# Layer-one routing with 8-column counting products, fused steps from threshold to list, and a different share of expert work per round

## What is computed

```python
def _moe_ref(x, w_gate, w1, w2):
    N, D = x.shape                       # 3072 tokens, 512 features
    E = w_gate.shape[1]                  # 8 experts
    cap = N // E                         # 384 tokens each
    logits = x @ w_gate
    order = np.argsort(-logits.flatten())
    assigned = -np.ones(N, dtype=np.int64)
    counts = np.zeros(E, dtype=np.int64)
    for idx in order:                    # best (token, expert) pair first
        tok, e = (int(idx) // E, int(idx) % E)
        if assigned[tok] >= 0 or counts[e] >= cap:
            continue
        assigned[tok] = e
        counts[e] += 1
...
    for e in range(E):
        mask = assigned == e
        h = np.maximum(x[mask] @ w1[e], 0.0)     # w1[e]: 512 x 1024
        out[mask] = h @ w2[e]                    # w2[e]: 1024 x 512
```

## Time and profile before

| | us |
|---|---|
| median of 3 runs | 844.89 |
| lowest and highest | 844.82, 845.41 |
| profiled execution | 845.31 |
| its span | 843.5 |

### The profile page before, as it was taken

One profiled execution on the slowest core, in us unless ns is written; L12 is line 12 of the kernel. 1 busy time (PEld: TensorE's weight loads), 2 busy tenths in 40 slices (PEclk: granted clock), 3 DMA queues, 4 the chain that ended last, 5 costly groups with the idle time before them and its releaser, 6 DMA issues.

```text
span 843.5 us, 15049 instructions
## 1 busy us (share of the span) xinstructions
PE 797.3 (95%) x4960; PEld 510.3 (61%) x4960; DVE 465.2 (55%) x2146; ACT 228.2 (27%) x681; POOL 216.0 (26%) x313
## 2 busy tenths in 40 slices
PE   5999997797899999999999999999999999999996
PEld 5878785786345445454554545555577686777762
DVE  6989895677777676776767677607049100000000
ACT  5878785421102121121211212121111111110101
POOL 6888973001021020302102021120300321211110
PEclk9999999899999999999999999999999999999999
DMA  9976650436071440706225071446987999898983
GB/s 260 279 235 208 222 151 2 181 129 224 6 262 51 142 170 3 283 26 222 90 75 211 26 261 51 148 164 240 361 321 293 414 372 348 308 338 310 332 318 105
DMA packets 64506, 171.66 MB, mean 204 GB/s; under 512 B 5585, under 2 KB 5585, under 8 KB 64449
## 3 DMA queue, kind: packets, MB, share of 16 engines
q1 hardware_dynamic: 54512, 143.70, 48.3%
q0 software_dynamic: 6480, 20.91, 6.8%
q10 hardware_dynamic: 3456, 6.29, 1.9%
HBM read 148.41 MB, written 22.81 MB: 203 GB/s over the span
## 4 chain that ended last, share of the span: by engine, by line
PE 75%; DVE 14%; DMA 4%; issue 3%; POOL 3%; ACT 1%; DVEq 0%; SPq 0%; POOLq 0%; ACTq 0%
PE bank L1433 16%; PE bank L1447 16%; PE bank L1575 11%; PE bank L1557 11%; DVE junk L987 4%; PE bank L1301 4%; PE bank L1328 3%; PE bank L1310 3%; PE bank L1506 2%; DMA weights<-in_moe_w 1%; PE bank L1298 1%; PE bank L1422 1%; PE bank L1633 1%; PE bank L1601 1%; PE bank L1646 1%
## 5 line engine op out<-in xcount | busy, mean ns | idle before, releaser
L1433 PE MATMUL bank<-features,weights 128*128 128x384 f32 x512 | 182.3, 497 | 0.6 <-ACT features L749 0.6
L1447 PE MATMUL bank<-weights 128*128 128x512 f32 x384 | 179.2, 602 | 0.0
L987 DVE TENSOR_SCALAR_CACHE_REDUCE junk<-Vt,cand 128x192 bf16<-128x192 f32 x376 | 136.1, 410 | 4.8
L1433 PEld LDWEIGHTS bank<-features,weights 128*128 128x128 f32 x512 | 89.5, 191 | 50.6 <-issue 5.6
L1557 PEld LDWEIGHTS bank<-x2T,weights 128*128 128x128 f32 x896 | 102.2, 192 | 5.9 <-issue 5.9
L1557 PE MATMUL bank<-x2T,weights 128*128 128x128 f32 x896 | 102.6, 275 | 0.0
L1447 PEld LDWEIGHTS bank<-weights 128*128 128x128 f32 x384 | 66.8, 190 | 58.5 <-issue 56.5
L1575 PE MATMUL bank<-weights,h2T 128*128 128x512 f32 x224 | 98.8, 593 | 0.4 <-ACT h2T L816 0.4
L1147 DVE SCALAR_TENSOR_TENSOR o<-bank,gate,x 128x512 f32<-128x512 f32 x14 | 10.5, 751 | 154.5 <-PE bank L1575 154.4
L754 ACT ACTIVATE weights<-bank 128x384 f32<-128x384 f32 x64 | 31.4, 490 | 141.4 <-PE bank L1433 141.4
L1575 PEld LDWEIGHTS bank<-weights,h2T 128*128 128x128 f32 x224 | 41.3, 190 | 46.5 <-issue 46.5
(11 more groups left out here) (324 smaller groups left out, 1048.3 us busy)
## 6 DMA issues: line engine op xcount, KB each, us to landing
weights<-in_moe_w SPq DMA_DIRECT2D x52, 2048.0 KB, 9.6
vw<-in_vwin SPq DMA_DIRECT2D x16, 576.0 KB, 4.9
qc<-in_qT SPq DMA_DIRECT2D x16, 384.0 KB, 5.3
kc<-in_kT SPq DMA_DIRECT2D x16, 384.0 KB, 5.8
vc<-in_vT SPq DMA_DIRECT2D x16, 384.0 KB, 7.4
x_rows<-xr SPq DMA_DIRECT2D x24, 256.0 KB, 2.2
y_rows<-weights ACTq DMA_DIRECT2D x24, 256.0 KB
weights<-x_rows,gidx POOLq DMA_INDIRECT x24
```

The source lines that it names most:

```text
L987: ins = ve.tensor_scalar(junk[:, c, :], Vt[:, :], cand[:, c:c + 1].bitcast(fp32), 0.0, ALU.is_ge, ALU.add, accum_out=cnt[:, c:c + 1])
L1433: ins = mm(HB[r % 2][:, 0:CAP], w1[:, c, 128 * r:128 * r + 128], xgT[:, c, :], start=(c == 0), stop=(c == KC - 1))
L1447: ins = mm(YB[j % 2][:, :], hT[:, r, 128 * j:128 * j + 128], w2[:, r, :], start=(r == 0), stop=(r == FC - 1))
```

## The change

- **Narrow products.** The count product streams the 8 columns of cnt, where it streamed them 16 times over (128). The threshold product streams 8 columns, the base products 2. The two base products now accumulate into one result of two columns (rowt has a zero column ahead, so that the second one is shifted), where VectorE added two results.
- **Fewer steps from threshold to list.** The comparison with tau and the multiply by revE are one step, the comparison with oneM and the multiply by V another. The steps to e_i move behind the row copy. The part of the rank that does not need the base is made before the base product is waited for, and the base is read as a scalar out of PSUM. The comparison that leaves oneE as a mask moves behind sel.
- **The first list's copies move ahead.** In search(1) alone, folded is copied before the first comparison and gidx right after it.
- **A signal for each tile.** xg_in becomes xg_in0 to xg_in2. TensorE waits for a tile's own.
- **Window 1's table.** The rounds get 111 units (6 in the second round, then 9, 6, 6 five times) where they got 90, the step behind the threshold product 16 for 15, the step behind the base product 22 for 28: 161 units for 145. The other windows' tables are as before.

```diff
@@ first_max @@
                 o.step(ve.tensor_reduce(m, src, X, ALU.max))
+                first_list = isinstance(ids_of, int) and ids_of == 0
+                if first_list:
+                    fold_out(ids_of)
                 o.step(ve.tensor_tensor(tmp, src, bc(m, shape, 2), ALU.is_equal))
-                if ids_of is not None:
+                if first_list:
+                    ids_out(ids_of)
+                elif ids_of is not None:
                     fold_out(ids_of)
...
-                if ids_of is not None:
+                if ids_of is not None and not first_list:
                     ids_out(ids_of)
@@ search @@
-                o.step(ve.tensor_scalar(oneE[:, :], TAU[:, 0:E], tau[:, :], None, ALU.is_equal))
-                o.step(ve.tensor_tensor(oneE[:, :], oneE[:, :], revE[:, :], ALU.mult))
+                o.step(ve.scalar_tensor_tensor(out=oneE[:, :], in0=TAU, scalar=tau[:, :], in1=revE[:, :],
+                                               op0=ALU.is_equal, op1=ALU.mult))
                 o.step(ve.tensor_reduce(oneM[:, :], oneE[:, :], X, ALU.max))
-                o.step(ve.tensor_scalar(oneE[:, :], oneE[:, :], oneM[:, :], None, ALU.is_equal))
+                o.step(ve.scalar_tensor_tensor(out=t1[:, :, :], in0=bc(oneE[:, :], full, 1), scalar=oneM[:, :], in1=V[:, :, :],
+                                               op0=ALU.is_equal, op1=ALU.mult))
+                o.step(ve.tensor_reduce(mx[:, :], t1[:, :, :], X, ALU.add))
...
+                ve.tensor_copy(rowt[:, 1:3], scn[:, :, NT - 1]).then_inc(s["rows_ready"], 1)
+                o.step(ve.scalar_tensor_tensor(out=rank[:, :, :], in0=scn[:, :, :], scalar=float(-BIG_SLOT), in1=GT[:, :, :],
+                                               op0=ALU.add, op1=ALU.subtract))
                 o.step(ve.tensor_scalar(e_f[:, :], oneM[:, :], -1.0, float(E), ALU.mult, ALU.add))
...
+                dve.wait_ge(s["base_mm"], ph + 1)
                 for h in range(2):
-                o.step(ve.tensor_copy(base[:, 0:2], BAS[:, 0:2]))
-                o.step(ve.tensor_copy(base[:, 2:3], BASN[:, 0:1]))
-                o.step(ve.tensor_tensor(base[:, 1:2], base[:, 1:2], base[:, 2:3], ALU.add))
...
+                    o.step(ve.scalar_tensor_tensor(out=rank[:, h, :], in0=rank[:, h, :], scalar=BAS[:, h:h + 1],
                                                    in1=GT[:, h, :], op0=ALU.add, op1=ALU.mult))
...
                 o.step(ve.tensor_scalar(sel[:, :], slot[:, :], CAP - 0.5, None, ALU.is_lt))
+                o.step(ve.tensor_scalar(oneE[:, :], oneE[:, :], oneM[:, :], None, ALU.is_equal))
@@ room @@
                 if w == 1:
-                    return [0] + [0, 0, 6] + [6] * (ROUNDS - 3) + [15, 28, 4, 8]
+                    return [0] + [0, 6] + [9, 6, 6] * 5 + [16, 22, 4, 8]
@@ load_x @@
-                if j == 0:
-                    pe.wait_ge(s["xg_in"], 16 * CT * (k + 1))
+                pe.wait_ge(s[f"xg_in{j}"], 16 * (k + 1))
@@ window @@
-                    mm(CNT, same_e[:, :], cnt[:, :].unsqueeze(1).to_broadcast([128, WIDE // 8, 8]),
-                       start=True, stop=True).then_inc(s["cnt_mm"], 1)
+                    mm(CNT, same_e[:, :], cnt[:, :], start=True, stop=True).then_inc(s["cnt_mm"], 1)
...
-                mm(BAS, tri[:, :], rowt[:, :], start=True, stop=True)
-                mm(BASN, ones_bf[:, :], rowt[:, :], start=True, stop=True).then_inc(s["base_mm"], 1)
+                mm(BAS, tri[:, :], rowt[:, 1:3], start=True, stop=False)
+                mm(BAS, ones_bf[:, :], rowt[:, 0:2], start=False, stop=True).then_inc(s["base_mm"], 1)
```

45 lines of the change are left out of this document (21 added, 24 removed).

## The result

The kernel before took 845.15 us beside it, the changed kernel 858.81 us (medians of four runs each): a ratio of 1.0154, 95% interval 1.0124 to 1.0183. I had predicted 841.5 us and a range of 838.5 to 844.4. The profiled execution took 857.25 us with a span of 855.4, 11.9 us more than the 843.5 of before.

A forecast was written before the change was run, and what follows sets the result against it. TensorE was taken as the bound (75% of the chain of waits, VectorE 14%). Windows 0, 1 and 2 gain 1.2, 3.25 and 0.7, windows 3 to 7 lose 1.75: 844.89 - 3.4 gives 841.5 us, range 838.5 to 844.4.

The forecast's parts named there:

- rival (c): Windows 3 to 7: gather of x, asked for earlier, lands 1.0 us late each (846.5) or 1.3 (848.0); chance 7%.
- 1.3 us in hand: Windows 3 to 7: gather lands 3.7 us after issue, so 1.3 us remain before the first tile of x is used.
- No wait for it shows before: Layer one's gather of x: argument against lateness, as the kernel before shows no wait for it.
- rival (b): Regrouping costs what it brings: 0.65 us lost in each of windows 3 to 7, window 1's fold later; 844.0; chance 12%.
- the expert's number 1 us later: Window 0, behind tau: number comes 1 us later, weights still have 5 us in hand with ten for 2 MB.
- The regrouping: Windows 3 to 7: 16 shifted units make more rounds short; 0.35 us lost per window, 1.75 in five.
- +0.2 with 16 units more: Window 1: takes 161 units, not 145, yet lasts only 0.2 us longer, saving later windows 3.45 us of products.
- 25.5 us to the threshold product: Window 1, from count 3 (9.9 us after V) to the threshold product: 25.5 us, where it was 26.1.
- Window 0: First search window: narrow rounds give 0.6 us, the stretch to the list 0.55; V comes 1.2 us earlier, rounded.
- rival (a): Windows 1 to 7: narrow product also saves 0.025 us where TensorE is late, 2.0 us in all; 839.5; chance 18%.
- Window 2: Third search window: TensorE's idle time before the base product and before V shrinks; 0.7 us gained.
- I shift everything rigidly: Behind window 7: products run without a gap worth naming, so everything there moves earlier by what was won.

The follow-up runs named there:

- e3: Changed kernel with the expert's number (e_f, e_i) worked out early, right after the maximum of oneE: 850.67 us, ratio 1.0041 to the kernel before.
- e4: Changed kernel with the second weight load held in every window until the three tiles of x have landed: 852.11 us, ratio 1.0065 to before.
- e1: Changed kernel with window 1's table as it was before, all else of the change kept: 842.35 us, ratio 0.9945 to before.
- e5: Changed kernel with 16 units less in window 2, so later items stand in their former rounds: 842.68 us, ratio 0.9960 to before.
- e11: Changed kernel with window 1's old table and fewer fillers in window 0 (11 for 14, 16 for 22): ratio 0.9891 to before.
- e8: Changed kernel with fillers added in TensorE's idle time around V of window 1: 857.68 us, ratio 1.0118 to before.
- e9: Changed kernel with the expert's number early and TensorE waiting for all three tiles of x before the first: 858.6 us, ratio 1.0145 to before.
- e2: Kernel before with window 1's new table and nothing else changed: 871.62 us, ratio 1.0302 to before.

## Why the prediction was wrong, point by point

**The gather: right mechanism, but at 7% a rival and not the forecast.** Rival (c) named the place, the queue and the point of decision. The step that failed is "1.3 us in hand": it took the landing time of 3.7 us from window 0, whose second load is held back until the rows are there, and applied it to windows in which 4 MB go ahead. From issue to use the changed kernel took 6.7, 6.4, 6.1, 6.4 and 6.2 us in windows 3 to 7. The row for layer two, 6.0 us under full traffic, stood beside it and was the nearer one; by it rival (c) was the forecast. "No wait for it shows before" spoke of a kernel that asked 3.6 us later (8.4 us after V), and was no evidence on one that asks earlier. The waits of windows 3 to 7 add up to 6.3 us, inside rival (c)'s own 5.0 to 6.5. That the kernel went 11 us past (c)'s 848.0 comes from what follows. Part of it is rival (b)'s: both rivals held at once, and each had been priced alone.

**The weights' later issue was costed at nothing outside window 0.** The prediction had the expert's number 1 us later; it is 1.6 (e_i 3.45 us behind the threshold product, 1.83 before). It checked only that the weights still land in time (right: no product of layer one waited for them), and did not ask what shares the queue with them. e3 shows it: with the number early the loss is 0.4% in place of 1.5%, since the gather then lies 10.8 us behind the load and not 8.4.

**The regrouping: right sign, too small.** In windows 3 to 7, the prediction had 0.73 us more idle time from short rounds (1.58 against 0.85), about 0.38 won elsewhere, 0.35 net. Without waits for x (e4) window 4 takes 51.28: 0.68 more than before and 1.31 more than e1. I add up TensorE's idle time by starts, that is, by how much a start lies behind its usual distance from the one before. Ahead of the count products it is 1.76 in e4, in the five rounds that the prediction had listed, 0.81 in before and 0.74 in e1, with two such rounds each. So the short rounds cost 0.95, not 0.73, and 0.27 is won elsewhere, not 0.38. That 0.2 "stays" before the base product was right (0.19 in before and in e4). In e1 that wait is gone too, since five first products stand ahead of it: under the old order the narrow and fused steps gain 0.63 a window (50.60 to 49.97), and the new order gives that away. Rival (b), at 12%, had 0.65 lost in each of these windows, and the 0.68 of e4 is that: its mechanism was right too.

**Window 1: the work is not free.** Predicted +0.2 with 16 units more; undisturbed it is +0.81 (e5 against before), and +2.13 in the changed kernel, where the clock's fall explains the rest. The fourth count comes 9.86 us after V in e5, as predicted (9.9), and 11.19 in the changed kernel with the fall in it. The part behind the threshold product is 1.27 shorter, near the predicted 0.8 to 1.2. What was wrong was the stretch between: 25.5 us to the threshold product, and 26.46 in e5. A round behind a TensorE-late one was to take 1.75, since VectorE would catch up; it takes 1.85, which is 0.4 to 0.5 over the stretch. The rest is a slip in the sum: thirteen rounds by the prediction's own lengths and its 0.35 at the end give 26.1, not 25.5. Against e1, with the old table and the same steps, window 1 pays 2.61 us for the 3.45 us of early work: only 0.84 is hidden.

**Window 0: the right total, in part by luck.** -1.42 against -1.2. Base product 3.54 us behind the threshold product (3.68 predicted), fold at 8.68 (8.9), and both bound by fillers, as e11 shows. But V gains only 0.26 us behind the threshold product (12.91 to 12.65), where 0.55 was predicted, and the stretch up to it gained 1.16 for 0.6, of which 0.37 is an early round that took 2.22 us before and 1.85 here. With e1's, e4's and e5's window 0, of the same code, the gain would be 0.85 to 0.66. The count at 0.05 where VectorE is late and 0 where TensorE is: right, rival (a) was false. The fused steps cost what was predicted: two with a scalar out of PSUM take 0.53 us (0.56).

**Window 2 and the end.** -0.87 without a wait for x (e4), against -0.7: right; the wait of 0.55 us took most of it. "I shift everything rigidly" was wrong: behind the last V the changed kernel won nothing of its 3.45 us. TensorE's idle stretches there over 0.25 us add up to 9.1 us, and to 5.6 in the kernel before: two more gather waits (0.94 and 1.46 us) and, in layer two, one wait for x of 2.22 us where the kernel before has 0.58. The last isn't shown to be the change's: it is 2.33 in e1 and 0.72 in e11, with the same order. Window 7's own share of the order comes on top.

**The clock: not considered.** The text had the clock at 1.00 throughout and no term for a fall. Three falls with 1.7 us of clock missing in each are in the profile of the changed kernel and not in that of before. The one in window 3 came behind the 2.23 us wait, as in e8, whose window 3 takes 55.03 us; behind e9's wait of 2.83 us there was none. The one in the attention is outside the change. For the one in window 1 the cause stays open.

As a whole: of 11.9 us in the profile, waits for the gather are 8.3 on TensorE's side (6.8 in windows 2 to 7 and 1.5 behind them), of which some part only replaces idle time that would have been there (windows 4 to 6 lie 0.6 to 0.9 us above e4's, with waits of 0.9 to 1.2); the order of items is 0.68 in each of windows 3 to 7 against before; the clock is 1.3 in window 1 and up to 1.7 in window 3; 1.7 is scatter ahead of window 0. I don't divide it further, since a wait, the round behind it and the clock's fall overlap.

## What to carry over

Moving work earlier in an order moves its inputs' deadline too: for each load that feeds the moved work, take issue to landing from a place with the same traffic on the queues, not from the quietest one. A step that sets off a DMA belongs in the sum twice, once for who needs the data and once for who shares the queue behind it. And when an item order is shifted as a whole, recount every place at which an engine waits, the ones outside the rounds too; that a row shows no wait today says nothing about a request made 3.6 us earlier. And before a window's total is called right, compare it among kernels with the same code there: here the same code took 46.72 to 47.48 us.

## What the runs showed of the hardware

An idle stretch of TensorE doesn't only cost itself. Around the 3.04 us of idle time behind the attention the granted clock went to 0.50 in twelve of twelve profiles, for 6.8 us (10.2 in e2's), and filling it, with the 1.5 us that follow, with products that nobody reads kept it at 1.00 in two of two. Behind waits for the gather in layer one of 2.2 to 2.8 us it fell in four of seven places (2.23 in the changed kernel, 2.71 and 2.40 in e2, 2.26 in e8; not behind 2.54 and 2.60 in e2, nor 2.83 in e9), with 1.7 us of clock missing each time. Over all fourteen profiles, behind V of window 0, TensorE has seventeen idle stretches of 2.1 to 2.9 us, whatever they wait for, and the clock fell at seven of them. One idle stretch of 3.27 us (e8) had a fall too. Behind shorter waits for the gather no row shows it. The Trainium skill, page "TensorE: Matmul & The Clock Gate", section "HAM oscillation — how this bites in real kernels", describes such falls by waits for the DMA that are longer than these; the traces agree that they occur, and show them at 2.13 to 2.71 us as well, though not each time. They may be one source of the spread of 4 to 9 us among runs of one kernel (e1's longest run has a mean clock of 0.987, its shortest 0.992); that isn't shown.

A gather of 128 rows takes 3.7 us from issue to use when little else is on the queues, 3.9 to 5.3 us to its landing when it is issued 10.8 us behind the first of two 2 MB loads (the first tile of windows 2 to 7 of e9), and 6.1 to 6.7 from issue to use when it follows that load by 8.4 us (windows 3 to 7 of the changed kernel).
